# A gated tile on one Trainium2 core: half of the gated units as seven half-width block products by Strassen's scheme

## The reference, cut to what matters

```python
qn, kn = q / (norm(q, axis=1) + 1e-6), k / (norm(k, axis=1) + 1e-6)   # q, k, v: 1 x 6016 x 256
a = softmax(kn.T @ qn / tau)                    # 256 x 256
x = v @ a                                       # 6016 tokens x 256
xn = x / sqrt(mean(x * x) + 1e-6) * rms_g
g, val = xn @ w_gate, xn @ w_val                # 256 -> 1536 each
y = (g * sigmoid(g) * val) @ w_out              # 1536 -> 256
h = y @ w_in                                    # 256 -> 2048
out = (h - tanh(h)) @ w_out2                    # 2048 -> 256
```

## Time and profile before

| | |
|---|---|
| median of 3 runs | 1172.43 us (1172.07 to 1173.29) |
| profiled execution, its own time | 1172.61 us |
| its span, first to last instruction | 1170.5 us |
| PE, DVE, ACT, POOL busy | 1166.0, 850.6, 366.5, 40.6 us |
| granted TensorE clock | 1.000 |

### The profile page before, as it was taken

How to read it: one execution, slowest core, us unless ns; L and a number is a source line. 1 busy time by engine, 2 the same in 40 slices (tenths; PEclk the granted TensorE clock), 3 DMA queues, 4 the chain that set the end, 5 groups by cost and what they waited for, 6 DMA issues and landing times.

```text
span 1170.5 us, 15889 instructions
## 1 busy us (share of the span) xinstructions
PE 1166.0 (100%) x5318; PEld 978.2 (84%) x5318; DVE 850.6 (73%) x1445; ACT 366.5 (31%) x592; POOL 40.6 (3%) x28
## 2 busy tenths in 40 slices
PE   9999999999999999999999999999999999999999
PEld 7888888888888888888888888888888888888998
DVE  6888675865966767677586586676767758658666
ACT  7866522321411421321232141142132123113122
POOL 4710000000000000000000000000000000000000
PEclk9999999999999999999999999999999999999999
DMA  9613120010011001002001001100100100100100
GB/s 372 212 56 107 37 36 1 1 32 4 0 18 18 0 7 29 0 0 36 0 0 31 5 0 18 18 0 4 31 0 0 31 0 0 19 1 1 18 1 14
DMA packets 102154, 33.91 MB, mean 29 GB/s; under 512 B 89200, under 2 KB 97520, under 8 KB 102128
## 3 DMA queue, kind: packets, MB, share of 16 engines
q1 hardware_dynamic: 101696, 33.05, 11.1%
q10 hardware_dynamic: 432, 0.52, 0.1%
HBM read 27.40 MB, written 6.16 MB: 29 GB/s over the span
## 4 chain that ended last, share of the span: by engine, by line
PE 99%; DMA 1%; SPq 0%; issue 0%; ACT 0%
PE ring L1114 51%; PE out_acc L1148 20%; PE y_acc L1148 16%; PE ring L1130 3%; PE out_acc L1098 2%; PE y_acc L1047 2%; PE y_acc L1057 1%; PE out_acc L1204 1%; DMA qk_in<-in_q_dram 1%; PE y_acc L1210 0%; PE out_acc L1212 0%; SPq L400 0%; PE y_acc L1114 0%; PE y_acc L1336 0%; PE y_acc L1212 0%; PE out_acc L1336 0%
## 5 line engine op out<-in xcount | busy, mean ns | idle before, releaser
L613 ACT ACTIVATE act<-ring 128x512 f32<-128x512 f32 (+1 forms) x333 | 196.3, 590 | 707.9 <-PE ring L1114 618.0
L1114 PE MATMUL ring<-y_hi,wl 128*128 128x512 f32 (+1 forms) x712 | 241.2, 385 | 0.0
L1148 PE MATMUL out_acc<-h_hi,wl 128*128 128x512 f32 x704 | 239.8, 389 | 0.0
L912 DVE TENSOR_TENSOR h_lo<-act,h_hi 128x512 fp32r<-128x512 f32 (+1 forms) x336 | 228.6, 681 | 10.9
L899 DVE TENSOR_TENSOR act<-ring,act 128x512 f32<-128x512 f32 (+1 forms) x141 | 94.9, 673 | 143.9 <-ACT act L613 143.8
L1114 PE MATMUL ring<-x_hi,wl 128*128 128x512 f32 (+1 forms) x576 | 186.4, 384 | 0.0
L908 DVE TENSOR_TENSOR act<-ring,act 128x512 f32<-128x512 f32 (+1 forms) x192 | 129.0, 672 | 77.9 <-ACT act L613 77.5
L1148 PEld LDWEIGHTS out_acc<-h_hi,wl 128*128 128x128 f32 x704 | 132.2, 188 | 27.5
L1114 PEld LDWEIGHTS ring<-y_hi,wl 128*128 128x128 f32 x712 | 133.5, 188 | 25.5
L1008 DVE CAST h_hi<-act 128x512 fp32r<-128x512 f32 (+1 forms) x308 | 129.7, 421 | 12.9
L1114 PE MATMUL ring<-y_lo,wl 128*128 128x512 f32 (+1 forms) x356 | 137.0, 385 | 0.0
(11 more groups left out here) (195 smaller groups left out, 1240.7 us busy)
## 6 DMA issues: line engine op xcount, KB each, us to landing
out_dram<-out_rows SPq DMA_DIRECT2D x88, 64.0 KB, 1.8
qk_in<-in_k_dram SPq DMA_DIRECT2D x9, 512.0 KB, 9.2
qk_in<-in_q_dram SPq DMA_DIRECT2D x9, 512.0 KB, 10.2
v_in<-in_v_dram SPq DMA_DIRECT2D x72, 64.0 KB, 2.2
w_in<-in_moe_w_out_dram SPq DMA_DIRECT2D x12, 256.0 KB, 3.0
w_in<-in_moe_w_in_dram SPq DMA_DIRECT2D x8, 256.0 KB, 3.3
w_in<-in_moe_w_gate_dram SPq DMA_DIRECT2D x6, 256.0 KB, 3.9
w_in<-in_moe_w_val_dram SPq DMA_DIRECT2D x6, 256.0 KB, 5.0
```

What stands on the lines that cost most here:

```text
L613: nc.scalar.activation(act[:, u % RING, 0:width], bank(t, name)[:, 0:width], func).then_inc(act_ready, 1)
L912: nc.vector.tensor_tensor(h_lo[:, u % RING, 0:width], act[:, u % RING, 0:width], f32(h_hi[:, u % RING, 0:width]), ALU.subtract).then_inc(h ...
L1114: ins = nc.tensor.matmul(bank(t, name)[:, 0:width], weights(c, w_part), (hi if part else lo)[:, c, 0:width], start=c == 0 and w_part and part,
L1148: ins = nc.tensor.matmul(acc[:, d, 0:width], down_weight(kind, f, d, w_part), (h_hi if part else h_lo)[:, u % RING, 0:width], start=f == 0 ...
```

## The change

In tiles 2 to 11 the six even gated units (0, 2, 4, 6, 8, 10) are computed in another way; tiles 0 and 1, the odd gated units and the hidden units stay. (Which channels a unit has is permuted: the even places take channels of the second half of gate and value, `gated_unit`.) For an even unit the 2 x 2 blocks are gate and value by the two chunks of input channels, and the two chunks by the two halves of the tile's columns. Eight block products would be 24 matmuls of 256 columns (the same columns as 12 of 512); the scheme makes seven, `FIRST_FOUR` and `LAST_THREE`, so 21 matmuls of 256 columns. Four of the seven use sums of x (`t_hi`, `t_lo`, made once a tile from hidden steps 11 to 14 of the tile before), four use sums of the weights.

- The sums of the weights are made in tile 1 (`sum_weights`, `cast_sums`, `split_sums`) and stored in a DRAM tensor `combined` with the plain parts: 1 MB per even unit. SBUF holds the blocks of three units; SP loads one (`load_sevens`) when the unit that used the place has all its products, and POOL copies what landed in place as fp32r (`mark_seven`, two copies of 128x1024), for which PE waits.
- DVE makes gate and value from the seven products by seven additions of 256 columns (`seven_sums`). The sigmoid then reads `gate_pair` in SBUF; POOL multiplies sigmoid and gate (`gate_seven`); DVE multiplies by the value (`seven_value`), in the middle of the next odd unit. ACT copies the first product out and makes the high part of units 0 to 10 (`cast_any`); DVE's low parts of two units go between the additions (`low_before`).
- The first four products take four banks of the ring. After them comes `down`, and then the last three: the first of them into the bank that it had before, the others into banks of the ring, or into `y_acc` in steps 0 and 2.

```diff
+def seven_order(gated, wide):
...
+    for p in range(gated):
+        if p % 2 == 0:
+            order += [(name, p) for name in ("own", "sum2", "sum3", "sum1")]
+        else:
+            order += [("gate", p), ("value", p)]
...
+        FIRST_FOUR = (("own", 0, (0, 0)), ("sum2", 4, 1), ("sum3", 6, 2), ("sum1", 7, 0))
+        LAST_THREE = (("own", 1, (1, 0)), ("sum1", 5, (1, 1)), ("sum2", 3, 3))
...
+            if name == "own":
+                return BY_GATE0
+            if name == "sum3":
+                return BY_VALUE1
+            if p < LAG:
+                return BY_U2 if name == "sum2" else BY_U4
+            return BY_VALUE0 if name == "sum2" else BY_GATE1
...
+                    sp.wait_ge(seven_full, sevens(t, 2 * (j - len(SEVEN_BLOCKS)), PRODUCTS, PRODUCTS))
...
+                sp.dma_start(landing[:, :, SEVEN_BLOCKS[n], :],
+                             combined[j].rearrange("p h s n -> p h (s n)")).then_inc(seven_loaded[n], 16)
...
+            with sp.Fori(SEVEN_FROM + 1, TILES - 3) as t:
+                for j in range(LOADS):
+                    load_sevens(t, j)
                 store(t - 1, TILE)
+                load_sevens(t, LOADS)
                 sp.wait_ge(v_turned, t)
                 load_v(t + 2, TILE)
...
+                for j in range(LOADS + 1, 2 * LOADS):
+                    load_sevens(t, j)
...
+            def mark_seven(t, j):
...
+                pool.wait_ge(seven_loaded[n], t * 32 + (16 * (j // len(SEVEN_BLOCKS) + 1) - 32 * SEVEN_FROM))
+                for low in range(2):
+                    nc.gpsimd.tensor_copy(wl[:, low, SEVEN_BLOCKS[n], :],
+                                          landing[:, low, SEVEN_BLOCKS[n], :]).then_inc(seven_ready, 1)
...
+                pool.wait_ge(act_ready, t * U + p + 1)
+                nc.gpsimd.tensor_tensor(buf, gate_pair[:, 0:width], buf, ALU.mult).then_inc(seven_gated, 1)
...
+            for t in range(SEVEN_FROM, TILES):
+                for j in range(SEVENS):
+                    gate_seven(t, 2 * j)
+                    ahead = j + len(SEVEN_BLOCKS)
+                    if t < TILES - 1 or ahead < SEVENS:
+                        mark_seven(t + ahead // SEVENS, ahead % SEVENS)
...
+            def seven_unit(t, p, width):
...
+                act_e.wait_ge(seven_full, sevens(t, p, PRODUCTS, OWN))
+                if p > 0:
+                    act_e.wait_ge(seven_gated, sevens(t, p))
+                nc.scalar.copy(gate_pair[:, 0:half], bank(t, ("own", p))[:, 0:half]).then_inc(own_copied, 1)
+                if p > 0:
+                    cast_any(t, p - 1, width)
+                act_e.wait_ge(seven_step, sevens(t, p, STEPS, BY_GATE1))
...
+                nc.vector.tensor_tensor(u2, of("sum2"), gate0, ALU.add).then_inc(seven_step, 1)
+                dve.wait_ge(seven_step, sevens(t, p, STEPS, BY_U2))
+                dve.wait_ge(seven_full, sevens(t, p, PRODUCTS, SUM3))
+                nc.vector.tensor_tensor(value0, of("sum3"), u2, ALU.add).then_inc(seven_step, 1)
+                dve.wait_ge(seven_full, sevens(t, p, PRODUCTS, SUM1))
+                nc.vector.tensor_tensor(gate1, of("sum1"), u2, ALU.add).then_inc(seven_step, 1)
+                dve.wait_ge(seven_step, sevens(t, p, STEPS, BY_U4))
+                nc.vector.tensor_tensor(value1, of("sum3"), gate1, ALU.add).then_inc(seven_step, 1)
+                low()
+                dve.wait_ge(seven_full, sevens(t, p, PRODUCTS, OWN_LAST))
+                nc.vector.tensor_tensor(gate0, last_of("own"), gate0, ALU.add).then_inc(seven_step, 1)
...
+                    if is_plain(t):
+                        gate_times(t, f, buf, width)
+                    else:
+                        gate_times(t, f, buf, width, lambda: seven_value(t, f - 1, width))
+                        if f == G - 1:
+                            low_unit(t, f - 1, width)
...
+                    if is_seven(t, f):
+                        seven_products(f, LAST_THREE, True)
```

More of the change, by code:

```diff
@@ L46, in bank_order @@
         order += [("gate", f), ("value", f)]
+    for f in range(wide):
+        order.append(("hidden", f))
+    return {name: n for n, name in enumerate(order)}
+def seven_order(gated, wide):
+    order = []
+    for p in range(gated):
[3 more added lines that the diff above has]
+            order += [("gate", p), ("value", p)]
     for f in range(wide):
@@ L298, in build, with is_plain, freed, sevens @@
         assert BANKS % RING == 0 and U % RING == 0
-        def before(t, name):
-            return t * BANKS + ORDER[name]
+        SEVEN_ORDER = seven_order(G, H)
+        SEVEN_BANKS = len(SEVEN_ORDER)
+        assert SEVEN_BANKS % RING == 0
+        PLAIN_AT = {}
+        for bank_name in SEVEN_ORDER:
+            if bank_name[0] in ("gate", "value", "hidden"):
+                PLAIN_AT[bank_name] = len(PLAIN_AT)
+        PLAINS = len(PLAIN_AT)
+        AT_NUMBER = {n: name for name, n in SEVEN_ORDER.items()}
+        BEFORE_SEVEN = SEVEN_FROM * BANKS
+        def is_plain(t):
+            return isinstance(t, int) and t < SEVEN_FROM
+        def before(t, name):
+            if is_plain(t):
+                return t * BANKS + ORDER[name]
+            return t * PLAINS + (BEFORE_SEVEN - SEVEN_FROM * PLAINS + PLAIN_AT[name])
+        def freed(t, name):
+            return before(t, name) + 1
+        def sevens(t, p, each=1, more=0):
+            return t * (SEVENS * each) + ((p // 2 - SEVEN_FROM * SEVENS) * each + more)
+        def is_seven(t, p):
+            return not is_plain(t) and p % 2 == 0
+        def gated_unit(t, p):
+            if is_plain(t):
+                return p
+            return G // 2 + p // 2 if p % 2 == 0 else p // 2
         def bank(t, name):
@@ L692, in tile @@
                             cast_x(t + 1, ahead, f - X_CAST)
+                        if f == T_CAST:
+                            cast_t(t + 1, ahead)
             first_tile()
-            with act_e.Fori(1, TILES - 2) as t:
+            tile(1, False)
+            with act_e.Fori(SEVEN_FROM, TILES - 2) as t:
                 tile(t, False)
@@ L1009, in split_unit, with beside @@
                     low_unit(t, u, width)
-                for f in range(G):
-                    gate_times(t, f, act[:, f % RING, 0:width], width)
-                    split_unit(f, before(t, ("value", f)) + 1)
+                def beside(f):
                     if f < KC:
@@ L1357, in _ @@
             tile(0, True, False)
-            with pe.Fori(1, TILES - 2) as t:
+            tile(1, False, False)
+            with pe.Fori(SEVEN_FROM, TILES - 2) as t:
                 tile(t, False, False)
```

290 lines of the change are left out of this document (272 added, 18 removed).

## The result

The changed kernel takes **1402.32 us** (median of 4 runs, 1401.4 to 1403.5) against 1172.86 in the same session (1172.07 to 1173.35): a ratio of 1.196, 95% interval 1.194 to 1.198, so 230 us slower. The forecast was 1378, range 1315 to 1440. The profiled execution took 1402.32 with a span of 1400.5.

What follows compares the result with a forecast made beforehand. PE bounded the kernel before (99% of the chain). Waits of 23.4 us a tile less 1.2 of matmuls gave 177.6 in tiles 2 to 9; 1172.6 + 177.6 + 10.5 + 12.2 + 4.5 + 0.5 = 1377.9, so 1378, range 1315 to 1440.

Steps and rivals of the forecast that it cites:

- Matmuls: Even gated units: 21 narrow matmuls take 2.52 us in place of 2.72, 0.20 saved each, 12 us in all.
- Unit 0 and unit 2: PE waits 0.98 at unit 1's gate, 0.64 at unit 2's fourth product, 2.54 at unit 3's gate.
- Unit 3's block, 3.4, and unit 5's, 10.65: Late block loads hold POOL's products; PE waits 3.4 us at unit 4's fourth product, 10.65 at unit 6's.
- the clock falls too: Rival: after the two long waits PE runs at the lower clock, about 40 us more, 1418; chance 0.30.
- the six matmuls of the gate after it add 1.28: Within the clock rival: unit 7's gate matmuls, after the long wait, run at the lower clock and add 1.28 us.
- The ports: POOL and DVE hinder each other at DVE's value product of unit 4: 0.5 us in 9 tiles, 4.5.
- Unit 11: Unit 11 and its finish: DVE and ACT have the last low part before PE comes to it, no wait.
- Units 8 and 10: Undisturbed units: DVE's chain takes 3.28 us against PE's own 2.44, so PE waits 0.84 each.
- Unit 4: PE waits 1.24 us at unit 5's gate for the bank that unit 4's fifth addition frees.
- unit 6: ACT's casts precede its copy, so the fifth addition is late and PE waits 2.29 us at unit 7's gate.
- the blocks do not hold POOL: Rival: blocks come in time, 3.4 and 10.65 fall away, about +6.8 us a tile, 1241; chance 0.10.
- PE stays the bound: Rival: DVE's chain fits into PE's work, so only the 12 us of matmuls remain, 1161; chance 0.03.

Runs made afterwards that it cites:

- run 4: Kernel before, with 21 narrow matmuls replacing 12 wide ones in even gated units of tiles 1 to 11, results not computed: 1163.01 us.
- run 1: Changed kernel with SP issuing the block for unit 8 before it waits for the turned v: 1334.0 us.
- run 5: Changed kernel with all three later block loads issued ahead of the v loads, the first also ahead of the stores: 1247.57 us.
- run 9: Changed kernel with POOL's product of gate and activation ahead of its block copies, all else kept: 1273.82 us.
- run 3: Changed kernel with DVE's two low parts behind the last three additions: 1408.76 us.
- run 8: Changed kernel with bf16 filler matmuls into the unused half of `out_acc` where PE waits longest: 1411.49 us.
- run 12: As run 10, with the block copies made by ACT and POOL only multiplying: 1189.67 us, ratio 1.015.
- run 11: As run 10, with POOL's product ahead of the copies: 1226.08 us.
- run 10: As run 5, with the products' banks reordered, sum2, own, sum3, sum1 for the first units: 1212.64 us.
- run 7: As run 5, with the four products' banks in another order and DVE's two lows behind the seven additions: 1218.26 us.

## Why the prediction was right, and where it was short

The time lies in the range, and the order of the stalls was the one written down. The moments of tile 4, counted from PE's first product (480.98):

| moment | forecast | measured |
|---|---|---|
| gate of unit 1 | 3.50 | 3.21 |
| fourth product of unit 2 | 7.94 | 7.64 |
| gate of unit 3 | 11.92 | 11.45 |
| POOL's copies of block 3 | 15.4 | 16.15 |
| fourth product of unit 4 | 20.47 | 20.88 |
| gate of unit 5 | 24.51 | 25.29 |
| SP issues block 4 | 30.35 | 31.56 |
| POOL's copies of block 4 | 35.25 | 37.37 |
| fourth product of unit 6 | 40.32 | 42.80 |
| gate of unit 7 | 45.41 | 47.48 |
| next tile | 117.4 | 120.5 |

- *Matmuls.* "0.20 saved" was 0.18 (run 4): 8 us instead of 12 in all, with the last tile's loss that the rows by the columns didn't show.
- *Unit 0 and unit 2*, waits of 0.98, 0.64 and 2.54: the moments came within 0.5 us, on the early side.
- *Unit 3's block, 3.4, and unit 5's, 10.65.* The mechanism is shown by runs 1, 5 and 9. The size was short: "I take 3.0 plus ... 4.9" for a landing. SP's issue at 491.40 and POOL's start at 497.13 are 5.7 apart, those at 512.54 and 518.35 are 5.8, and the page's median is 5.4. That is 0.8 to 0.9 on each of two chains, the first of which the waits behind it took up in part.
- *What the sum of waits hid.* I listed 3.4 and 10.65 as the price of two blocks. Run 1 showed that the second price comes back as another if only its block is moved, and run 3 that time won ahead of a block's wait is waited away at it. The sum was right for this kernel, but its terms could not be subtracted one by one.
- *The clock.* The rival "the clock falls too" came true in the profile (four windows at 0.50 to 0.66) and not in its price: not 40 us but about 10, as run 8 shows. 1402 lies between the sum's 1378 and this rival's 1418 and nearer the rival, so the time alone would not have told them apart. The step that failed there is "the six matmuls of the gate after it add 1.28": those of the gate of unit 7 (from 528.46) start 0.23 apart, at the full clock, and run 8 wins nothing between the fourth product of unit 6 and that gate. Behind the other wait, "1.3 of it shows" was 0.9. Still, this 1.2 us a tile was in no term of the forecast's sum.
- *The ports.* I took 4.5 us in 9 tiles. The value product met the copy in 9 tiles in the way I described, and lost not 0.5 but 0.7. In tile 4:

```profile
521.72 1.40 DVE L1212 TENSOR_TENSOR act<-w_in,act 128x512 f32<-128x512 f32 x1 [12.33 <-POOL act L725]
...
550.91 1.26 DVE L1352 CAST h_hi<-act 128x512 fp32r<-128x512 f32 x1
```

  The second row I had not foreseen: the cast of unit 11 (0.43 where nothing runs beside it) loses 0.8 to the copies of the block for the next tile. The Trainium skill (SBUF — State Buffer, Who interferes with whom) has both: a VectorE instruction with two inputs in SBUF contends with a GpSimd instruction that reads SBUF, a copy or cast can too, and whoever comes second waits. The trace agrees with the waiting; POOL's pair of copies in turn takes 2.49 instead of 2.02 when it meets one.
- *Unit 11*, "nothing": its down matmuls wait 0.74 for DVE's low part,

```profile
553.68 0.50 PE L1557 MATMUL y_acc<-h_hi,wl 128*128 128x512 f32 x1 [0.74 <-DVE h_lo L1256]
```

  which is most of the 1 us that the tile loses between the gate of unit 7 and its end.
- *Units 8 and 10*, 0.84 each: a pair of units takes 8.69 (528.46 to 537.15), forecast 8.80; with no wait it would be 7.98.
- *Unit 4*, 1.24, and *unit 6*, 2.29: from the fourth product to the next gate are 4.41 and 4.68, forecast 4.04 and 5.09. One was 0.4 short, by the clock, the other 0.4 long; that they cancel is luck.
- *Tile 10*, +10.5 and ports 0.5: +11.7. *Tile 11*, +12.2: +14.3. *Tile 1 and the prepared sums*, 0.5: -0.4, so the making of the weights' sums costs no time.

The miss of 24 us is thus about 3 us in each of eight tiles: landings 1.3, the clock 1.2, ports and unit 11 the rest, as far as they can be told apart; only the clock's part has a run of its own (run 8), and it falls partly on the same stretch as the landings'.

The other rivals: "the blocks do not hold POOL" asked for 1241, and run 5, in which they don't, took 1247.6, so its price was well made though its condition failed. "PE stays the bound" would have had 1161: run 4 has 1163, and no version with the additions on DVE came there.

## What to carry to other kernels

When matmuls are taken from a bound TensorE and vector work is added, ask of every queue what stands *behind* the new instruction, not only how long it takes: here one product behind one copy cost 128 us, more than ten times what the matmuls could save. Stalls that lie one behind another are not a sum, and a single fix can move the wait to the next block, as in run 1; move them all, or take the waiting instruction out of the queue. And put bulk copies where they do not slow the engine that sets the pace: the same copies moved from POOL to ACT gave back 23 us. Last, set the gain against the waits before building: 8 us in ten tiles are used up by 0.8 us of waits in a tile, and run 12, the best, still has 2.6.

## What was not expected of the hardware

- POOL copies of 128x1024 and DVE operations of two SBUF operands stop each other: 0.69 becomes 1.41 in 53 cases (run 11), and two lows of 1.28 become 2.16 (run 10). POOL's product does the same: two lows become 2.41 beside it (run 7). An addition with an operand in PSUM is not touched: the 152 of run 10 that begin during a copy take 0.35 to 0.43, as those beside nothing do.
- TensorE's clock fell to half (1.2 GHz) not only in the wait of 12 us but already behind the wait of 2.10, with waits of 0.53 and 0.35 ahead of it (493.00 to 496.00: 0.50). It did so behind the like wait in six of the eight full tiles, and not in the other two. In run 5, where the longest wait of a full tile is 2.2 to 2.5 us and most are 0.4 to 0.9, it did so in none, and the mean clock is 0.999. So the length of one wait does not tell.
- A narrow matmul with its own weight load gets hardly cheaper below 256 columns: 0.120 at 256, 0.111 at 192, where the columns alone would let it go down to three quarters.
